# Moving one reduction, one vector instruction and one wait at the seam between the attention stage and the gated layer of a fused kernel

## The reference

```
attention: mask[q,k] = bucket(q) == bucket(k)          (2 x 8 heads, 768 tokens, head 64)
           x = softmax(mask ? q k^T / 8 : -1e9) v      -> x is 1536 tokens x 512
gated:     xn = x / sqrt(mean(x*x) + 1e-6) * rms_g
           y  = (silu(xn @ w_gate) * (xn @ w_val)) @ w_out        (512 -> 1536 -> 512)
routed:    e  = argmax(y @ w_gate2); out = prob_e * sigmoid(y @ w_og)[e] * relu(y @ w1[e]) @ w2[e]
                                                       (8 experts, 512 -> 1024 -> 512)
```

## Time and profile before

| | |
|---|---|
| median of 3 runs | 797.71 us |
| the profiled execution | 797.35 us |
| its span | 795.5 us |
| PE busy in the span | 767.3 us (96%) |
| DVE / ACT / POOL busy | 501.4 / 375.2 / 316.9 us |
| mean granted clock of PE | 0.995 of full speed |

### The profile page before, as it was taken

How to read it: one execution, slowest core, us unless ns; L and a number is a source line. 1 busy time by engine, 2 the same in 40 slices (tenths; PEclk the granted TensorE clock), 3 DMA queues, 4 the chain that set the end, 5 groups by cost and what they waited for, 6 DMA issues and landing times.

```text
span 795.5 us, 14327 instructions
## 1 busy us (share of the span) xinstructions
PE 767.3 (96%) x4294; PEld 680.7 (86%) x4294; DVE 501.4 (63%) x983; ACT 375.2 (47%) x672; POOL 316.9 (40%) x340
## 2 busy tenths in 40 slices
PE   6899999999999999999999999999889999999995
PEld 5799899888888999999999988888768888778774
DVE  7999999999987643444433534454673647655540
ACT  5888888888886211101111234433423534553331
POOL 7877787788887543443333001111200201010110
PEclk9999999999999999999999999999999999999998
DMA  7888669658301221112110220032454567454410
GB/s 200 231 244 217 198 173 269 180 139 189 84 2 48 87 80 40 40 58 61 40 40 0 92 80 27 26 133 80 147 151 141 163 219 242 159 199 175 148 45 22
DMA packets 53717, 96.84 MB, mean 122 GB/s; under 512 B 6841, under 2 KB 21189, under 8 KB 53656
## 3 DMA queue, kind: packets, MB, share of 16 engines
q1 hardware_dynamic: 48648, 84.90, 36.3%
q10 hardware_dynamic: 2768, 4.87, 2.4%
q0 software_dynamic: 2240, 6.31, 2.0%
HBM read 58.51 MB, written 21.04 MB: 100 GB/s over the span
## 4 chain that ended last, share of the span: by engine, by line
PE 83%; DVE 8%; issue 3%; POOL 2%; ACT 2%; DMA 1%; ACTq 0%; POOLq 0%; DVEq 0%
PE ps_t L1061 13%; PE ps_s L924 12%; PE ps_s L1111 11%; PE ps_t L1131 11%; PE ps_t L924 6%; PE ps_t L877 6%; DVE pT_l L1485 3%; PE ps_o L924 3%; PE ps_p L924 3%; PE ps_s L864 2%; PE ps_s L863 2%; DVE negmax L1467 2%; PE ps_s L1122 2%; PE ps_o L892 1%; PE ps_o L894 1%
## 5 line engine op out<-in xcount | busy, mean ns | idle before, releaser
L697 POOL TENSOR_SCALAR probs<-probs,rden,alone 128x768 f32<-128x768 f32 x96 | 93.5, 987 | 35.4 <-DVE rden L1479 35.3
L1485 DVE TENSOR_TENSOR pT_l<-ps_t,pT_h 128x384 fp32r<-128x384 f32 x192 | 97.4, 548 | 5.7 <-ACT pT_h L1221 4.7
L806 POOL DMA_INDIRECT out_dram<-rows_out,rows_in x16 | 23.0, 1440 | 194.0 <-ACT rows_out L1382 184.1
L924 PE MATMUL ps_s<-xn,w_h 128*128 128x384 f32 x384 | 97.5, 334 | 0.0
L1211 ACT ACTIVATE probs<-ps_s,negmax 128x768 f32<-128x768 f32 x96 | 87.0, 906 | 19.1 <-DVE negmax L1467 18.2
L1221 ACT ACTIVATE pT_h<-ps_t 128x384 fp32r<-128x384 f32 x192 | 85.3, 490 | 16.5 <-PE ps_t L877 15.6
L1467 DVE TENSOR_REDUCE negmax<-ps_s 128x1 f32<-128x770 f32 x96 | 90.7, 946 | 3.1 <-PE ps_s L864 2.3
L1656 DVE TENSOR_TENSOR expert_w<-piece,expert_w 128x2048 f32 (+1 forms) x32 | 72.1, 2288 | 31.8 <-ACT expert_w L1350 26.6
L877 PE MATMUL ps_t<-ident,probs 128*128 128x128 f32 x576 | 87.5, 282 | 4.8 <-DVE pT_l L1485 2.6
L1131 PE MATMUL ps_t<-expert_w,hidT_h 128*128 (+1 forms) x256 | 82.1, 402 | 2.1 <-DVE hidT_l L1811 1.4
L877 PEld LDWEIGHTS ps_t<-ident,probs 128*128 128x128 f32 x576 | 63.1, 141 | 24.4 <-DVE pT_l L1485 9.7
(11 more groups left out here) (252 smaller groups left out, 1707.5 us busy)
## 6 DMA issues: line engine op xcount, KB each, us to landing
piece<-in_moe_w_dram SPq DMA_DIRECT2D x32, 1024.0 KB, 5.8
routed<-filler SPq DMA_DIRECT2D x52, 257.0 KB, 4.6
k_a<-qk_h SPq DMA_DIRECT2D x28, 192.0 KB
rows_in<-routed ACTq DMA_DIRECT2D x17, 257.0 KB, 2.7
rawv<-in_v_dram SPq DMA_DIRECT2D x8, 384.0 KB, 6.0
w_raw<-in_moe_w_gate_dram SPq DMA_DIRECT2D x12, 256.0 KB, 3.1
w_raw<-in_moe_w_val_dram SPq DMA_DIRECT2D x12, 256.0 KB, 3.4
wo_raw<-in_moe_w_out_dram SPq DMA_DIRECT2D x12, 256.0 KB, 2.7
```

Of the source, the lines that this page charges most:

```text
L697: nc.gpsimd.tensor_scalar(pr, pr, rden[:, j:j + 1], alone[:, j:j + 1], ALU.mult, ALU.add).then_inc(norm_done, 1)
L924: mm = nc.tensor.matmul(unit_banks[tg][w][:, 0:G], a_[par][:, w, c, :], xn_at(tg, part, c), start=(n == 0), stop=(n == 3 * C - 1))
L1485: nc.vector.tensor_tensor(pT_l[u % 4][:], ps_t[kt % 2][:, 0:G], pT_h[u % 4][:].bitcast(F32), ALU.subtract).then_inc(low_ready, 1)
```

## The change

On POOL, `split_w(1, 1)` no longer waits for DVE's last addition and its last low part; the wait for the low parts stands behind it, ahead of `split_wo(0)`. On PE, the sum over partitions of group 3 moves ahead of the value unit of group 2, right behind that of group 2, and the turn of the reciprocals moves from inside the gate unit of group 3 to ahead of it; a wait for x_done that has already been passed is added. On DVE, one low part (number 10) moves from behind add_last(1) to ahead of it.

```diff
@@ gpsimd @@
             pool.wait_ge(x_done, 4 * PAIRS)
-            pool.wait_ge(last_added, 2)
-            pool.wait_ge(xnl_dve, len(DVE_LOWS))
             run(split_w(1, 1))
             pool.wait_ge(summed, TG)
             pool.wait_ge(xnh_made, XNH_DONE)
+            pool.wait_ge(xnl_dve, len(DVE_LOWS))
             split_wo(0)
             split_wo(1)
@@ tensor @@
             run(unit(0, 0, 2, 0, True))
             pe.wait_ge(x_done, 4 * PAIRS)
             sum_squares(2)
+            sum_squares(3)
             run(unit(0, 0, 2, 1, True))
-            sum_squares(3)
-            last_gate = unit(0, 0, 3, 0, True)
-            some(2, last_gate)
             turn_rinv(1)
-            run(last_gate)
+            pe.wait_ge(x_done, 4 * PAIRS)
+            run(unit(0, 0, 3, 0, True))
             pe.wait_ge(factors_row, 2)
             run(unit(0, 0, 3, 1, True))
@@ vector @@
             add_last(0)
-            lows_xn(DVE_LOWS[8:10])
+            lows_xn(DVE_LOWS[8:11])
             add_last(1)
-            lows_xn(DVE_LOWS[10:12])
+            lows_xn(DVE_LOWS[11:12])
             invert((2, 3))
             rows_of_factors(1)
```

## The result

The changed kernel takes 803.07 us (median of 7 runs, 801.62 to 804.82) beside 798.31 us for the kernel before (7 runs, 796.06 to 801.09). The ratio is 1.0055, 95% interval 1.0039 to 1.0070: 4.4 us slower, between 3.1 and 5.6. (The two medians by themselves are 4.8 us apart, which lies inside that interval.) The profiled execution took 803.83 us with a span of 801.9.

A forecast was written before the change was run, and what follows sets the result against it. PE was taken as the bound, without idle time from 260 to 451 us. A 3.09 us stall less 0.12 saved gave +2.97 on the 797.71 median: 800.7 us, range 798.6 to 803.0.

The forecast's parts named there:

- PE bound, nothing won back: From 260 to 451 us PE has no idle time, so any time it stands still is never won back.
- DVE's list alone makes PE wait 0.2 us: One more low ahead of add_last(1) delays it 0.53 us; PE stalls 0.21 before sum_squares(3), +0.1 with PE's saving.
- POOL's two instructions delay DVE by 2.88 us, 0.77 and 2.11: Early w_h (0.77) and w_l (2.11), reading SBUF, hold up DVE's lows ahead of add_last(1).
- own time less 0.27: A POOL instruction reading SBUF delays DVE's two-input lows by its own duration less about 0.27 us.
- two meetings: At 244.74 and 248.92 us, lows met a POOL square and a POOL addition; DVE was delayed 0.56 and 0.75.
- Rival A: At the seam w_h and w_l don't block DVE: stall 0.21 us, time 797.8, not slower; chance 0.15.
- Both go in ahead of add_last(1), the gap is 3.09 us: w_h and w_l run before DVE's second addition, ending 263.92; PE idles 260.97 to 264.06 before sum_squares(3).
- The saving of 0.12 on PE: PE's reordered sums, value unit and gate unit take 7.05 us from 260.97 instead of 7.17.
- rival B: PE's granted clock also falls behind the gap, costing 1.72 us more: 4.69 in all, 802.4; chance 0.16.
- The 4.00 us at 0.57 in the earlier trace: Behind PE's 2.43 us wait at 578.96 the granted clock was 0.57 over 4.00 us, a loss of 1.72.
- The rest stays covered: ACT's root, the reciprocal, hT tiles, w_l and split_wo(0) behind the seam all keep more than 1 us of room.

The follow-up runs named there:

- e1: The changed kernel with POOL's two waits (last_added, DVE's lows) back ahead of split_w(1, 1), PE's and DVE's new orders kept; ratio 0.9993 to the kernel before.
- e7: The changed kernel with only w_h early on POOL, w_l waiting again for DVE's last addition and last low; ratio 1.0027 to the kernel before.
- e9: The changed kernel with POOL's two waits back and add_last(1) moved up behind the first of DVE's last four lows; ratio 1.0002 to the kernel before.
- e2: The kernel before with POOL's part of the change alone, PE's and DVE's old orders kept; ratio 0.9995 to the kernel before.
- e3: The changed kernel with 18 unused 128x384 matmuls added between PE's two sums to fill the gap; ratio 1.0036 to the kernel before.
- e11: The changed kernel again, unaltered, for a third trace, on another chip; a single execution without a ratio, seam 4.78 us longer than before.
- e4: The changed kernel with DVE's old order (two lows, add_last(1), two lows) back; ratio 1.0046 to the kernel before.
- e8: The changed kernel again, unaltered, for a second trace; ratio 1.0062 to the kernel before, seam 6.35 us longer.
- e10: The changed kernel with DVE's old order once more, for a second trace, on another chip; a single execution without a ratio, seam 4.26 us longer than before.

## Why the prediction was right in its mechanism and short in its size

- *PE bound, nothing won back.* Right. The delay of the seam reaches the end: the seam is 6.11 us longer, and the two profiled executions are 6.48 apart.
- *DVE's list alone makes PE wait 0.2 us.* Right: gap 0.2 in e1. With PE's order it was to cost 0.1 in all, and the seam of e1 is 0.35 longer, because of the two terms on PE below.
- *POOL's two instructions delay DVE by 2.88 us, 0.77 and 2.11.* Right: three lows took 4.54 instead of 1.67, a delay of 2.87; e7 gives 0.79 for w_h, which leaves 2.08 for w_l. The rule "own time less 0.27", taken from two meetings with other POOL instructions, held for both. Rival A, no collision, fell. Its evidence, a low of 0.65 us beside a one-input POOL instruction that ran 0.23 us more, says nothing against the rule: 0.23 is less than 0.27.
- *Both go in ahead of add_last(1), the gap is 3.09 us.* Right, to the last digit.
- *The saving of 0.12 on PE.* Wrong: e9 shows a seam of the old length. I had taken 0.56 for each of two sums side by side; together they take 1.23, and the 0.11 saved on the gate unit is gone.
- *Missing: what it costs PE to begin again.* A sum (three matmuls of the kernel, six in the trace) takes 0.80 us behind a gap (e1, e2, e7) and adds 0.56 in the flow. A gap without a fall of the clock makes the seam 3.2 us longer (3.21 by e1's pieces, 3.25 in e3) and not 2.97.
- *The clock.* This is the term that was mis-sized. The forecast gave it nothing and rival B 1.72 us with a chance of 0.16, since PE had run dense units ahead of the gap. It fell all five times behind gaps of 2.6 and 3.1 us, and cost 1.5 to 3.1 us. The 4.00 us at 0.57 in the earlier trace rows stood behind a wait of 2.43 us; that row deserved more weight, and the dense units ahead of the gap were no reason to set it aside.
- *The time.* What happened is rival B. The kernel before was at 797.71 us when the forecast was made and at 798.31 in this comparison, so the increases are what to compare: 3.0 forecast, 4.7 for rival B, 4.4 measured (3.1 to 5.6). The range of 798.6 to 803.0 means 0.9 to 5.3 more and holds 4.4 only because rival B was counted in; as an absolute time 803.07 would lie just outside. By its first trace the change loses 6.1 us at the seam, by e11's 4.8. That the three traces differ by 1.6 us in the clock's term is part of the distance to 4.4; the rest isn't settled.
- *The rest stays covered.* Right: PE had no other wait between the gap and 451 us.

## What to carry to other kernels

A wait on an engine that is idle anyway may be what keeps it out of another engine's way. Before you remove such a wait on GpSimd, look whether the freed instructions read SBUF while VectorE runs instructions with two inputs there. If so, add the freed instructions' own time, here less about 0.27 us each, to whatever waits for VectorE. Moving a consumer up to its producer and loading that producer are each harmless here and cost 4.4 us together, so work out again, with both in, how much room every wait has. Where TensorE would stand still for 2.6 us, as here, count the clock as well: 1.5 to 3.1 us on top of the gap. Dense matmuls in the gap, of no use otherwise, avoided it (e3).

## What the runs showed of the hardware that was not expected

- A POOL instruction that was waiting went in between two DVE instructions that stood back to back, in each of the seven traces of e2, e3, e4, e8, e10, e11 and the change: w_h (1.41 us) behind add_last(0), w_l (2.52 to 2.56) behind the first low. DVE did not keep its turn. An instruction of DVE with one input in SBUF, the reciprocal beside w_l, was not held up.
- POOL's instruction of one input (w_h) delays DVE like one of two: 0.79 us for 1.04.
- The slow stretch behind the same gap of 3.1 us cost 2.86, 3.10 and 1.53 us in three traces of one kernel.
- Behind a gap of 1.0 us the clock stayed at 1.00 (e7, one trace), behind 2.6 us it fell (e4, e10). The length of one gap is not the whole of it: in the trace of the change the clock is 0.57 from 577.50 to 581.50, and from 565 to 577.5, among small matmuls, PE had waited 0.73 us at most at a time.
